# Pad of 128 bytes ahead of the first expert's weights, and five steps of VectorE in another order

## The reference

```python
p_packed = sm_attn(p, k, v)            # 32 rows per head look at 576 tokens
out = sm_attn(q, p_packed, p_packed)   # 576 tokens look at 32 packed rows

rms = np.sqrt(np.mean(x * x, axis=-1, keepdims=True) + 1e-06)
xn = x / rms * rms_g                   # first expert, 512 -> 1536 -> 512
g, val = xn @ w_gate, xn @ w_val
x = (g * (1.0 / (1.0 + np.exp(-g))) * val) @ w_out

h = x @ w_in                           # second expert, 512 -> 2048 -> 512
out = (np.maximum(h, 0.0) + alpha * np.minimum(h, 0.0)) @ w_out
```

## Time and profile before

| | us |
|---|---|
| median of 3 runs (1592.49 to 1593.76) | 1593.41 |
| profiled execution, whole time | 1591.07 |
| its span, first to last instruction | 1589.3 |
| TensorE matmuls busy | 1566.7 (99% of the span) |
| TensorE weight loads busy | 1323.5 (83%) |
| VectorE busy | 750.1 (47%) |
| ScalarE busy | 447.7 (28%) |
| GpSimd busy | 183.5 (12%) |

### The profile page before, as it was taken

One profiled execution on the slowest core, in us unless ns is written; L12 is line 12 of the kernel. 1 busy time (PEld: TensorE's weight loads), 2 busy tenths in 40 slices (PEclk: granted clock), 3 DMA queues, 4 the chain that ended last, 5 costly groups with the idle time before them and its releaser, 6 DMA issues.

```text
span 1589.3 us, 25626 instructions
## 1 busy us (share of the span) xinstructions
PE 1566.7 (99%) x10326; PEld 1323.5 (83%) x10326; DVE 750.1 (47%) x1279; ACT 447.7 (28%) x849; POOL 183.5 (12%) x132
## 2 busy tenths in 40 slices
PE   8999999999999999999999999999999999999998
PEld 3889889898898989889988888888888888888887
DVE  5755554645555455554543434343444334343333
ACT  4444344444534444342211111111111111111111
POOL 2700000000000000007451001010101001010000
PEclk9999999999999999999999999999999999999999
DMA  9302112021210302003400001010100001010000
GB/s 354 99 16 78 46 45 67 12 78 45 78 46 1 107 16 76 16 16 148 146 3 27 26 0 53 0 53 0 46 7 26 26 14 39 0 53 0 27 0 27
DMA packets 42737, 76.15 MB, mean 48 GB/s; under 512 B 2208, under 2 KB 19616, under 8 KB 42656
## 3 DMA queue, kind: packets, MB, share of 16 engines
q1 hardware_dynamic: 37472, 65.55, 12.0%
q10 hardware_dynamic: 5184, 9.44, 1.6%
HBM read 56.11 MB, written 18.87 MB: 47 GB/s over the span
## 4 chain that ended last, share of the span: by engine, by line
PE 91%; DVE 4%; ACT 1%; issue 1%; DMA 1%; SPq 0%; ACTq 0%; DVEq 0%
PE psum L566 29%; PE psum L567 28%; PE psum L568 28%; PE psum L698 3%; DMA gv_sb<-w_gv 1%; DVE h_lo L1197 1%; DVE act_sb L1194 1%; ACT h_hi L956 1%; DVE sum L1072 1%; DVE m_lo L1144 1%; PE psum L586 1%; PE psum L600 0%; PE psum L660 0%; PE psum L648 0%; PE psum L667 0%
## 5 line engine op out<-in xcount | busy, mean ns | idle before, releaser
L1230 DVE TENSOR_TENSOR h_lo<-g,h_hi 128x512 fp32r<-128x512 f32 x144 | 124.3, 863 | 468.1 <-ACT h_hi L983 468.1
L983 ACT CAST h_hi<-g 128x512 fp32r<-128x512 f32 x144 | 89.3, 620 | 649.8 <-PE psum L568 579.5
L566 PE MATMUL psum<-an_hi,m_hi 128*128 128x288 f32 x768 | 238.0, 310 | 7.4 <-DVE sq L1102 4.3
L566 PE MATMUL psum<-h_hi,ow_hi 128*128 128x288 f32 x768 | 234.0, 305 | 0.5 <-DVE h_lo L1197 0.5
L567 PE MATMUL psum<-h_hi,ow_lo 128*128 128x288 f32 x768 | 227.2, 296 | 0.0
L567 PE MATMUL psum<-an_hi,m_lo 128*128 128x288 f32 x768 | 226.7, 295 | 0.0
L568 PE MATMUL psum<-h_lo,ow_hi 128*128 128x288 f32 x768 | 226.1, 294 | 0.0
L568 PE MATMUL psum<-an_lo,m_hi 128*128 128x288 f32 x768 | 225.8, 294 | 0.0
L566 PEld LDWEIGHTS psum<-h_hi,ow_hi 128*128 128x128 f32 x768 | 144.1, 188 | 34.7 <-issue 34.0
L566 PEld LDWEIGHTS psum<-an_hi,m_hi 128*128 128x128 f32 x768 | 144.1, 188 | 31.7 <-issue 16.9
L1197 DVE TENSOR_TENSOR h_lo<-act_sb,h_hi 128x288 fp32r<-128x288 f32 x192 | 110.7, 576 | 115.4 <-ACT h_hi L956 115.4
(11 more groups left out here) (139 smaller groups left out, 2376.8 us busy)
## 6 DMA issues: line engine op xcount, KB each, us to landing
k_sb<-k_t SPq DMA_DIRECT2D x16, 576.0 KB, 5.0
q_sb<-q_t SPq DMA_DIRECT2D x8, 1152.0 KB, 6.6
y_mid<-y_sb SPq DMA_DIRECT2D x16, 576.0 KB, 3.5
xs_raw<-y_mid SPq DMA_DIRECT2D x9, 1024.0 KB, 5.2
out_t<-o_sb ACTq DMA_DIRECT2D x36, 256.0 KB, 2.0
v_sb<-v_s SPq DMA_DIRECT2D x8, 1024.0 KB, 6.4
gv_sb<-w_gv SPq DMA_DIRECT2D x4, 1536.0 KB, 18.8
w_raw_front<-w SPq DMA_DIRECT2D x2, 2560.0 KB, 12.9
```

Of the source, the lines that this page charges most:

```text
L566: nc.tensor.matmul(dst, w_hi, hi, start=start, stop=False)
L983: nc.scalar.copy(h2_hi[:, f % 2, :], g32[:, f % 2, :]).then_inc(g_hi_done, 1)
L1230: nc.vector.tensor_tensor(h2_lo[:, s, :], g32[:, s, :], h2_hi[:, s, :].bitcast(F32), ALU.subtract).then_inc(g_lo_done, 1)
```

## The change

A pad is put ahead of `m_hi`, so that `m_at` has the remainder of `gv_at` by 256. Five steps change their place in the two tables of VectorE:
- `norm1` of batches 1 to 7 goes from ahead of the multiply of f = 4 to behind it, `probs0` from ahead of the multiply of f = 1 to behind it, and `weigh0` from behind `sums1` to ahead of it, both in half 1;
- of batch 0, `weigh1` goes from behind the subtraction of f = 3 to between multiply and subtraction, and `mean1` from ahead of the multiply of f = 5 to between multiply and subtraction of f = 4. There it stands ahead of `norm1` of batch 1.

```diff
@@ -54,11 +54,11 @@
 }
 DVE_PLACES = {
     (0, "between", 2): ["max0", "max1"], (0, "between", 3): ["norm0"],
-    (0, "within", 4): ["norm1"], (0, "between", 5): ["turn_a1"], (0, "within", 7): ["packed"],
+    (0, "after", 4): ["norm1"], (0, "between", 5): ["turn_a1"], (0, "within", 7): ["packed"],
     (0, "between", 8): ["turn_s0", "gram"], (0, "after", 9): ["shift0"], (0, "between", 9): ["turn_s1"],
     (0, "after", 10): ["shift1"],
-    (1, "between", 0): ["sums0"], (1, "within", 1): ["probs0"], (1, "between", 1): ["turn_p0", "fold0"],
-    (1, "between", 2): ["sums1", "weigh0"], (1, "after", 3): ["probs1"], (1, "between", 3): ["fold1"],
+    (1, "between", 0): ["sums0"], (1, "after", 1): ["probs0"], (1, "between", 1): ["turn_p0", "fold0"],
+    (1, "between", 2): ["weigh0", "sums1"], (1, "after", 3): ["probs1"], (1, "between", 3): ["fold1"],
     (1, "after", 4): ["turn_p1"], (1, "between", 4): ["weigh1"],
     (1, "within", 6): ["means"], (1, "between", 6): ["fold2"], (1, "between", 7): ["newton"],
     (1, "between", 8): ["fold3"], (1, "within", 10): ["split0"], (1, "between", 10): ["fold4"],
@@ -76,7 +76,7 @@
 }
 DVE_FIRST = {
     (0, "within", 0): ["fold3"], (0, "after", 1): ["sums1"], (0, "between", 1): ["probs1"], (0, "after", 2): ["turn_p1"],
-    (0, "between", 3): ["weigh1"], (0, "within", 5): ["mean1"], (0, "between", 7): ["newton1", "normed1"],
+    (0, "after", 3): ["weigh1"], (0, "after", 4): ["mean1"], (0, "between", 7): ["newton1", "normed1"],
     (0, "within", 10): ["split1"],
 }
 ACT_FIRST = {
@@ -151,6 +151,8 @@
         max2, sum2 = place("max2", small), place("sum2", small)
         rcp2 = place("rcp2", small)
 
+        same_rows = 256
+        cursor[0] += (gv_at - cursor[0]) % same_rows
         m_at = cursor[0]
         m_hi = place("m_hi", [P, NF1, GROUPS, GV], F32R)
         m_lo_at = cursor[0]
```

## The result

The changed kernel takes 1564.32 us, median of four runs (1561.99 to 1564.40); the kernel before took 1592.95 us beside it (1591.62 to 1593.76). The ratio is 0.9818, with a 95% interval of 0.980 to 0.9835: 28.6 us less, 1.8%. The forecast was 1565.9 us, 27.5 us less.

A forecast was written before the change was run, and what follows sets the result against it. TensorE was taken as the bound, by matmul pace in the second expert and with waits for VectorE before it. Gains of 14.8 + 9.9 + 2.8 = 27.5 us took 1593.41 to 1565.9 us, range 1562.5 to 1575.0.

The forecast's parts named there:

- Part 1: Second expert: with the pad, front matmul steps fall from 233.3 to 226.7 ns; -14.8 us net, between -14.2 and -15.8.
- the stalls at the first down steps: Second expert, 8 later tiles: first down step waits 0.07 to 0.2 us for ScalarE's output copies; +1.0 us in all.
- three slots at 288 columns: First expert's `h_hi`/`h_lo` slots, 1152 bytes apart: twelve down matmuls 1.59, 1.62, 1.59 us, so odd multiples of 256 suffice.
- Part 2: Batches 1 to 7, moved VectorE steps remove TensorE waits; -9.9 us, bounds -8.4 and -11.2.
- (a): Batches 1 to 7: `probs0` behind the multiply of f = 1 gains 0.56 us a batch at the first Gram matmul.
- this wait: First Gram matmul's wait for the fold's splits (idle 0.26 us) stays, so VectorE sets the gain there.
- (b): Batches 1 to 7: `weigh0` ahead of `sums1` removes the 0.62 us idle before the next fold; 0.86 us a batch.
- (c): Batches 1 to 7: `norm1` behind the multiply of f = 4 gains 0; if its cover went, 0.1 to 0.3 us lost.
- the second rival: Pushed-back `sums1` makes a new wait in batches 1 to 7; up to 6.0 us lost, 1571.9 us; chance 0.12.
- Part 3: Batch 0, once: moving `weigh1`, `mean1` and `norm1` shortens waits before the mean and transposes; -2.8 us, between -2.0 and -3.2.
- The rival that the addresses do nothing: Second expert: region or distance, not the remainder by 256, separates front from back steps; 1580.7 us; chance 0.10.
- the one on the other side: Second expert: an odd multiple of 256 is worst, front steps slow to 246.7 ns; 1609.6 us; chance 0.02.

The follow-up runs named there:

- `e3_pad384`: Changed kernel with a pad of 384 bytes instead of 128; twelve front matmuls of the second expert take 2.72 us, as in the changed kernel.
- `e6_probs0_back`: Changed kernel with `probs0` ahead of the multiply of f = 1 again; a batch takes 94.267 us against 93.481.
- `e7_weigh0_back`: Changed kernel with `weigh0` behind `sums1` again; a batch takes 94.376 us against 93.481.
- `e8_norm1_back`: Changed kernel with `norm1` ahead of the multiply of f = 4 again; a batch differs by 0.02 us.
- `e2_order_only`: Changed kernel without the pad, so only the moved VectorE steps against the kernel before; 1577.87 us, ratio 0.991 to the kernel before.
- e4: Changed kernel with a pad of 64 bytes instead of 128 (number inferred from the text's order); twelve front matmuls of the second expert take 2.79 us.
- e10: Changed kernel with ScalarE making all four output copies of a second-expert tile before sending any, last tile unchanged; second expert 783.22 us, 0.87 less.
- e13: Changed kernel with a pad of 224 bytes instead of 128 (number inferred from the text's order); twelve front matmuls of the second expert take 2.80 us.
- `e12_all`: Changed kernel with copies ahead of sends, fillers at two early waits, and one GpSimd subtraction cut into four; 1562.50 us, ratio 0.981 to the kernel before.
- `e1_pad_only`: Kernel before with the pad of 128 bytes alone, VectorE's old order kept; 1578.30 us, ratio 0.9909 to the kernel before.
- `e11_fillers`: Changed kernel with filler matmuls added at two early TensorE waits in the first expert's first tile; median 1563.38 us.

## Why the prediction was right, point by point

**Part 1, the addresses.** -14.8 forecast, -14.9 measured. But for the stalls at the first down steps, all steps fell to 226.7 ns, the steps out of order behind each change of region went with them, and the stall came, 0.87 us in all for the 1.0 assumed. The step of the argument that carried it was the earlier trace rows: three slots at 288 columns, with 0.03 us between them, showed that an odd multiple of 256 is as good as an even one, and `e3_pad384` and the changed kernel bear it out at 512. The Trainium skill ("SBUF — State Buffer", section "Who interferes with whom") gives TensorE two independent read ports, and has it wait for nobody. Whether TensorE waits for other engines was not tested here; but moving operand and weights don't come free of each other: 2.80 against 2.72 us for the same twelve matmuls, by their addresses alone. The measurement decides.

**Part 2, (a), was too small.** 0.56 us a batch forecast, 0.79 measured (`e6_probs0_back`). The timeline of the changed kernel, VectorE, beside the first two of the earlier trace rows:

```profile
276.57 0.27 DVE L1078 RECIPROCAL rcp<-sum 128x18 f32<-128x18 f32 x1
276.76 0.40 DVE L1196 TENSOR_TENSOR act_sb<-act_sb,psum 128x288 f32<-128x288 f32 x1
277.07 0.75 DVE L1083 TENSOR_TENSOR e<-e,rcp 128x576 f32<-128x576 f32 x1
277.73 0.46 DVE L1199 TENSOR_TENSOR h_lo<-act_sb,h_hi 128x288 fp32r<-128x288 f32 x1
...
278.79 1.25 DVE L1146 TENSOR_TENSOR m_lo<-psum,m_hi 128x512 fp32r<-128x512 f32 x2
```

and TensorE, fold, Gram product, next fold, in the changed kernel

```profile
275.75 1.09 PE L700 MATMUL psum<-gv_sb,pp_tg 64*32 64x512 f32 x16
...
280.19 1.21 PE L662 MATMUL psum<-a,gram_sb 128*128 128x288 f32 x4
...
282.92 1.09 PE L700 MATMUL psum<-gv_sb,pp_tg 64*32 64x512 f32 x16
```

and the two folds of the kernel before (its Gram product is in the earlier trace rows):

```profile
279.01 1.09 PE L698 MATMUL psum<-gv_sb,pp_tg 64*32 64x512 f32 x16
...
287.83 1.09 PE L698 MATMUL psum<-gv_sb,pp_tg 64*32 64x512 f32 x16
```

Counted from the fold, the multiply starts at 1.01 us; before it was 280.82 - 279.01 = 1.81. That is 0.80 earlier, not 0.68: the forecast let it start where `probs0` had, at 1.13, but it starts 0.19 behind the reciprocal where `probs0`, which reads it, had started 0.30 behind. The other 0.11 is in `probs0`: the forecast let the next instruction start a whole duration behind it, and it starts 0.66 behind. So the subtraction comes 0.77 earlier and the splits of the fold, which set the Gram product, 0.78: they ended 284.08 - 279.01 = 5.07 us after the fold, and now 4.29. The Gram product follows 0.15 us after their end in both kernels, and it starts 0.26 us behind the matmul ahead of it (279.93), where 0.13 is the step. So the forecast was right that this wait is what is late next, and that VectorE sets the gain there; it was wrong that the list would still show it, since the matmul ahead is recorded until 280.22 and no idle time is seen. From fold to Gram product it is now 4.44 us, before 5.22: 0.78 less.

**(b) and (c) held.** From the Gram product to the next fold it is 2.73 us, before 3.60: 0.87 less, 0.86 forecast, and 0.90 by `e7_weigh0_back`. No wait took its place: `sums1`, pushed back, runs at 282.61, and nothing of TensorE is late for it, so the second rival is out. `norm1` is worth nothing in the batches, as forecast (`e8_norm1_back`). Part 2 was 11.6 us, where 9.9 was forecast; that is outside its bounds of 8.4 and 11.2.

**Part 3 depends on how GpSimd and VectorE meet.** -2.8 forecast, -1.9 in the changed kernel's profile, a little outside the bounds of 2.0 and 3.2. In `e2_order_only`, whose first tile starts at the same time as that of before, it is 52.13 - 49.28 = 2.85. Its timeline, VectorE and TensorE, beside the earlier trace rows:

```profile
46.21 0.76 DVE L1102 TENSOR_TENSOR sq<-psum,a 128x576 f32<-128x576 f32 x1
...
47.00 1.17 DVE L1104 TENSOR_TENSOR sq<-sq 128x288 f32<-128x288 f32 x1
...
48.47 0.65 PE L667 MATMUL psum<-sq,mean_w 128*128 128x288 f32 x2
```

and that of the changed kernel, whose first tile starts 1.8 us later:

```profile
49.01 0.76 DVE L1104 TENSOR_TENSOR sq<-psum,a 128x576 f32<-128x576 f32 x1
...
49.80 1.20 DVE L1106 TENSOR_TENSOR sq<-sq 128x288 f32<-128x288 f32 x1
...
51.06 0.75 PE L669 MATMUL psum<-sq,mean_w 128*128 128x288 f32 x2 [0.37 <-DVE sq L1106]
...
55.47 1.09 PE L602 MATMUL psum<-ident,a_sb 128*128 128x128 f32 x8 [0.48 <-DVE a_sb L1038]
```

The product starts at 46.21 in the first (46.3 was forecast) and the mean has no wait. In the second, product and mean come 2.8 and 2.6 us later, with a start only 1.8 later, and both places keep a wait. Ahead of them `probs1` of this tile, beside GpSimd, takes 1.84 us in the changed kernel and 1.16 in `e2_order_only`. L1106 takes 1.17 to 1.20 us in both, where it takes 0.46 in the later batches, without a split of GpSimd beside it. In the seven kernels whose code for this tile is that of the changed kernel and whose clock fell in the start (first tile at 35.2 to 36.2 us: the changed one, e3, e4, e6, e7, e10, e13), it takes 49.44 to 50.80 us. The mean has no wait in e7 and e13 (49.45 and 49.44); e6, like `e12_all` (50.82), has a further wait of 0.4 us at the start of a chunk. When GpSimd's splits meet VectorE is what differs between them, as far as the traces show. So the term's size is known to some 0.7 us only, and a term of the forecast that hangs on one meeting of two engines was given too narrow a range.

**The sum.** 14.8 + 9.9 + 2.8 = 27.5 forecast; 14.9 + 11.6 + 1.9 = 28.4 measured, and 28.6 between the medians. That the sum came out within 1.1 us is in part luck: part 2 gave 1.7 us more and part 3 0.9 less than forecast, each outside its own bounds. The median is 1.6 us under the 1565.9 forecast: 1.1 by the gain, and 0.5 because the kernel before ran at 1592.95 beside it and not at 1593.41. The rival that the addresses do nothing is excluded by `e1_pad_only`, the one on the other side by `e3_pad384`.

## What to carry to other kernels

Where TensorE is the bound, measure the distance from start to start of the same matmul with operands in different places: here the place of the weights against the moving operand, by 256 bytes, was worth 3% of every step of 512 columns, for 128 bytes of pad (2.80 against 2.72 us for twelve). On an engine that runs in order, put the instruction for which the critical engine waits ahead of those that only become due later, and work out the new times from start distances, not from whole durations. Once steps get faster, look at what was just hidden: here ScalarE's copies, which should not stand behind the sends.

## What the runs showed of the hardware that was not expected

- Weights and moving operand of an fp32r matmul with 512 columns: 226.7 ns a step with the same remainder by 256 bytes, 233.3 with any other tried (64, 96 and 128 off, the same cost for each).
- The granted clock of TensorE fell to 1.2 GHz within the first 35 us of one execution and stayed at 2.4 in another with the same waits of 1.34 and 1.24 us; it made a fold of 1.95 us last 3.31. It fell in the ten profiles whose first six matmuls took 4.73 us or more, and not in `e11_fillers`, where they took 5.49 and the waits were filled.
- One two-input subtraction of 4.59 us on GpSimd makes VectorE's last 4.76 instead of 0.46 us. The Trainium skill ("SBUF — State Buffer", section "Who interferes with whom") says that the two share a read port for a second input; the traces agree. Beside four pieces of 1.3 to 1.5 us VectorE's took 1.53 and 1.04 us.
